# Row fetches from part of an expert loop, a gate product with its operands swapped, and four first tiles

## The reference

```python
x = attn_out.transpose(0, 2, 1, 3).reshape(B * S, H * D)          # 1536 x 512
logits = x @ w_gate
noisy = logits + np.log1p(np.exp(x @ w_noise)) * noise             # first mixture
top2 = np.argpartition(-noisy, 2, axis=1)[:, :2]                   # second: argmax(x @ w_gate)
...
h = np.maximum(x[mask] @ w1[e], 0.0)
out[mask] += top2_w[mask, k, None] * (h @ w2[e])                   # second: out[mask] = gate_w * ye
```

## Time and profile before

| | |
|---|---|
| three runs | 977.11, 982.68, 984.29 us, median 982.68 |
| the profiled execution | 984.25 us, its span 982.4 |
| busy | PE 857.7, PEld 727.2, DVE 601.8, ACT 356.4, POOL 412.4 us |
| mean granted clock of TensorE | 0.948 of full speed |
| stores of result tiles, both mixtures | 44 |
| chain that ended last | `DMA x_sb<-ys,pos 1%; POOL x_sb L568 1%; DVE x_sb L1133 0%; POOLq L53 0%` |
| L817, a reduction of 768 contiguous values to one, mean | 953 ns |
| ys<-stage 1024 KB, xs<-stage 512 KB, median to landing | 7.5, 5.5 us |

### The profile page before, as it was taken

One profiled execution on the slowest core, in us unless ns is written; L12 is line 12 of the kernel. 1 busy time (PEld: TensorE's weight loads), 2 busy tenths in 40 slices (PEclk: granted clock), 3 DMA queues, 4 the chain that ended last, 5 costly groups with the idle time before them and its releaser, 6 DMA issues. The chain is left out here.

```text
span 982.4 us, 17214 instructions
## 1 busy us (share of the span) xinstructions
PE 857.7 (87%) x4650; PEld 727.2 (74%) x4651; DVE 601.8 (61%) x1109; ACT 356.4 (36%) x597; POOL 412.4 (42%) x282
## 2 busy tenths in 40 slices
PE   4899999999984679999999999999566999999970
PEld 3788888888874568888888888887345888888860
DVE  5899999999986744444444444444475444444432
ACT  2677777777874114211111111101240344332000
POOL 3010101101040789643434343408747899885004
PEclk9999999999998598999999999999795999999995
DMA  6577659658685568442524252416674678773107
GB/s 146 125 205 203 148 156 242 181 120 219 187 295 199 176 251 257 169 164 91 165 88 168 89 167 94 162 65 209 205 231 171 213 249 252 231 248 109 43 33 257
DMA packets 100201, 171.46 MB, mean 175 GB/s; under 512 B 35600, under 2 KB 37648, under 8 KB 100176
## 3 DMA queue, kind: packets, MB, share of 16 engines
q1 hardware_dynamic: 66992, 82.79, 28.6%
q10 hardware_dynamic: 26944, 67.90, 21.4%
q0 software_dynamic: 6240, 20.45, 6.4%
HBM read 98.18 MB, written 53.48 MB: 154 GB/s over the span
## 5 line engine op out<-in xcount | busy, mean ns | idle before, releaser
L532 POOL TENSOR_TENSOR wring<-stage,wring 128x1024 f32 (+1 forms) x124 | 293.0, 2402 | 195.6 <-ACT wring L711 171.0
L711 ACT ACTIVATE wring<-stage 128x1024 f32 (+1 forms) x120 | 125.3, 1059 | 419.1 <-POOL wring L532 190.2
L1346 PE MATMUL bank<-wring,xT_hl 128*128 x352 | 144.0, 409 | 5.2 <-DVE xT_hl L1042 5.2
L1363 PE MATMUL bank<-wring,hT_hl 128*128 x352 | 142.7, 405 | 3.2 <-DVE hT_hl L1068 3.2
L1075 DVE COPY work<-bank 128x512 f32<-128x512 f32 x44 | 30.5, 693 | 181.0 <-PE bank L1365 171.3
L1348 PE MATMUL bank<-wring,xT_hl 128*128 x352 | 139.8, 397 | 0.0
L1347 PE MATMUL bank<-wring,xT_hl 128*128 x352 | 139.2, 395 | 0.0
L1365 PE MATMUL bank<-wring,hT_hl 128*128 x352 | 138.6, 394 | 0.0
L1364 PE MATMUL bank<-wring,hT_hl 128*128 x352 | 138.1, 392 | 0.0
L1056 DVE TENSOR_SCALAR work<-bank 128x512 f32<-128x512 f32 x88 | 60.9, 692 | 106.7 <-PE bank L1348 106.7
L516 POOL TENSOR_TENSOR wring<-raw,ones 128x192 fp32r<-128x192 f32 x32 | 15.5, 506 | 224.9 <-PE bank L1197 218.5
(11 more groups left out here) (173 smaller groups left out, 1356.3 us busy)
## 6 DMA issues: line engine op xcount, KB each, us to landing
stage<-in_moe_w_dram ACTq DMA_DIRECT2D x128, 512.0 KB, 3.9
wring<-wring SPq DMA_DIRECT2D x92, 192.0 KB
ys<-work SPq DMA_DIRECT2D x44, 256.0 KB, 3.6
work<-xs SPq DMA_DIRECT2D x40, 256.0 KB, 3.4
xs<-stage SPq DMA_DIRECT2D x7, 1024.0 KB, 4.8
ys<-stage SPq DMA_DIRECT2D x7, 1024.0 KB, 7.5
xs<-stage SPq DMA_DIRECT2D x7, 512.0 KB, 5.5
raw<-in_q_dram SPq DMA_DIRECT2D x16, 192.0 KB, 4.1
```

The lines of the kernel that those rows point to most:

```text
L532: nc.gpsimd.tensor_tensor(wring[:, bass.ds(at + DC * F, GW)], stage[:, at_stage(g, j), :], wring[:, bass.ds(at, GW)].bitcast(F32), ALU.sub ...
L711: nc.scalar.activation(wring[:, bass.ds(parity * SLOT + high_at(j), GW)], stage[:, j % STAGES, :], ACT.Copy).then_inc(w_high, 1)
L1346: mm(o, xT_hl[:, 0, c, :], wh, start=c == 0, stop=False)
L1363: mm(y_ps[:], hT_hl[:, 0, c, :], wh, start=c == 0, stop=False)
```

## The change

- The loads of constants on SP go behind the first head's puts.
- `lg_heads` is laid out with the head as the last index; both result buffers are cleared whole, a part in each round.
- `FIRST` is 4: four tiles are fetched directly from the tokens, at other places among the scatters.
- VectorE computes a table `need[m]`: for each token tile the number of sorted tiles whose results must be stored before its rows of the last expert can be fetched. `fetch_high` reads it before each fetch and waits for that many stores. For the first mixture eight tiles of rows go to `stage` and four to `work`, the latter after the last store.
- So that `stage` is free, ScalarE and POOL prepare only the first four pieces of the second mixture's expert 0 ahead; the other four are loaded while tiles are mixed, and VectorE splits them (`second_low`) as in the first mixture. Low parts 0 to 3 of expert 1 move into `sort_rows(1)`, ahead of scatter 7, the other four stay behind the scatters.
- The low rows are scaled by ScalarE; the gate weights are computed inside `experts`; the last scaling and the output stores are ScalarE's.
- The gate product has the turned rows as the stationary operand and the 8 gate columns moving; its result needs no turning back. Ten idle products more (`keep_busy(10)`) follow TensorE's counts.

```diff
-    FIRST = 3
+    FIRST = 4
@@ SP, start
+            sp.wait_ge(prep_ev, 2)
+            put(q_hl[0], D, D, qk_rest, 0)
+            put(k_lb[0], 0, D, qk_rest, D)
+            put_bits(0, 0)
+            load_qk(1)
             for r in range(2):
                 for at, w in ((D, moe_w_gate), (D + E, moe_w_noise)):
...
-                clear_y(0, i * share[0], share[0])
+                    clear_y(m, i * share[m], share[m])
...
-            clear_y(1, NTMIN[1], NT[1] - NTMIN[1])
+                clear_y(m, NT[m] - rest[m], rest[m])
@@ POOL
-                fetch_at = ((2, 6, 10), (2, 5, 8))[m]
+                fetch_at = ((1, 5, 7, 9), (1, 4, 5, 6))[m]
                 for t in range(TT):
                     if m == 1:
                         pool.wait_ge(mixed, t + 1)
+                        if t == 7:
+                            pool.wait_ge(w_low, (E + 1) * GRAN)
+                            low_part(E + 1, 1, range(GRAN // 2))
...
-            def fetch_rows(m):
-                pool.wait_ge(y_st, 16 * (T0[m] + NT[m]))
...
-                for t in range(TT):
-                    if t >= GOT:
-                        pool.wait_ge(mixed, m * TT + t - GOT + 1)
-                    fetch_one(y_got[t % GOT] if m == 0 else rows_of(t), m, TOPK[m] - 1, t, y_back[t % GOT])
+            def fetch_high(m):
+                for t in range(TT):
+                    if m == 0 and t >= EARLY:
+                        stored = pool.value_load(tiles_upto[0][0:1, E - 1:E], min_val=NTMIN[0], max_val=NT[0])
+                    else:
+                        stored = pool.value_load(need[m][0:1, t:t + 1], min_val=NTMIN[m] // E, max_val=NT[m])
+                    pool.wait_ge(y_st, stored * 16 + T0[m] * 16)
+                    pool.sem_inc(y_seen, 1)
+                    fetch_one(y_got(t) if m == 0 else rows_of(t), m, TOPK[m] - 1, t, y_back[t])
...
             pool.wait_ge(rt_tab, 1)
+            low_part(E, 0, range(GRAN // 2))
             fetch_low()
-            low_part(E, E % 2)
-            fetch_rows(0)
-            low_part(E + 1, 1, range(3))
+            pool.wait_ge(w_low, E * GRAN + GRAN // 2)
+            fetch_high(0)
             sort_rows(1)
-            low_part(E + 1, 1, range(3, GRAN))
+            low_part(E + 1, 1, range(GRAN // 2, GRAN))
@@ ACT
-            high_part(1, 0, E, 0, table(0, E - 2))
+            high_part(1, 0, E, 0, table(0, E - 2), range(GRAN // 2))
+            act.wait_ge(rt_gate, 1)
+            act.wait_ge(y_low, 16 * TT)
+            for t in range(TT):
+                nc.scalar.activation(x, x, ACT.Copy, scale=gatew[0][:, t:t + 1]).then_inc(low_scaled, 1)
             for t in range(TT):
                 act.wait_ge(rt_T, t + 1)
                 nc.scalar.activation(route_T(1, t), route_xT[t % 2][:], ACT.Copy).then_inc(rt_Tc, 1)
+                if t in (2, 4, 6, 8):
+                    act.wait_ge(mixed, t)
+                    load_piece(1, 0, GRAN // 2 + t // 2 - 1)
+            for j in range(GRAN // 2, GRAN):
+                second_high(j)
...
+            for t in range(TT):
+                act.wait_ge(y_back[t], 32)
+                nc.scalar.activation(x, x, ACT.Copy, scale=gatew[0][:, t:t + 1]).then_inc(out_rdy, 1)
+                act.wait_ge(out_rdy, t + 1)
+                act.dma_start(ot[t // QT, t % QT], x_sb[:, t // QT, t % QT]).then_inc(out_st, 16)
@@ DVE
-                vec.tensor_copy(tiles_upto[m][:], cum[0:1, :]).then_inc(rt_tab, 1)
+                link(vec.tensor_copy(tiles_upto[m][:], cum[0:1, :]))
+                link(vec.tensor_tensor(last_tiles[0:1], bc(last_seen[0:1], [1, TT, TT], 2), bc(steps128[0:1], [1, TT, TT], 1),
+                                       ALU.is_gt))
+                link(vec.tensor_reduce(last_seen[0:1], last_tiles[0:1], AX.X, ALU.add))
+                vec.tensor_scalar(need[m][:], last_seen[0:1], cum[0:1, E - 2:E - 1], None, ALU.add).then_inc(rt_tab, 1)
...
-                link(vec.tensor_scalar(x, x, gatew[0][:, t:t + 1], None, ALU.mult))
-                vec.scalar_tensor_tensor(out=x, in0=y_got[t % GOT], scalar=gatew[1][:, t:t + 1], in1=x,
+                vec.scalar_tensor_tensor(out=x, in0=y_got(t), scalar=gatew[1][:, t:t + 1], in1=x,
...
                 hT_split(0)
+                gate_weights(m)
@@ PE
-                    ins = mm(lgT_ps[t % 2], wg_sb[:, c, :], xt[:, c * P:(c + 1) * P], start=c == 0, stop=c == DC - 1)
-                ins.then_inc(rt_lgT, 1)
-            def turn_logits(t):
...
+                    ins = mm(lg_ps[:, t * E:(t + 1) * E], xt[:, c * P:(c + 1) * P], wg_sb[:, c, :],
+                             start=c == 0, stop=c == DC - 1)
+                ins.then_inc(rt_lg, 1)
```

161 lines of the change are left out of this document (78 added, 83 removed).

## The result

The changed kernel takes 973.26 us (median of 6 runs, 970.48 to 974.99) against 981.62 for the kernel before (6 runs, 977.11 to 984.29): a ratio of 0.9933, 95% interval 0.9909 to 0.9956. That is 8.4 us where the forecast summed up 19.8, though 973.3 lies inside the stated range of 956 to 975. The profiled execution took 972.41 with a span of 970.6, so against the profiled 984.25 the difference is 11.8.

The account below looks back on a forecast made before the run. TensorE is full inside both expert loops, so only the seams (start, first experts, between mixtures, end) can move. Terms sum to -19.8 from the profiled 984.25, giving 964.45, or 962.9 as a median; 8 in 10 range 956 to 975.

Parts of the forecast that it names:

- Start, -1.0: Kernel start: constants' loads behind the first puts bring TensorE's first scores 1.0 us earlier, bounds 0 and 3.9.
- Attention, -0.5: Attention: head sums laid out for contiguous reduction, 0.95 instead of 1.45 us, save 0.5; added clears cost nothing.
- First experts, -5.6 net of the chain: First mixture: a fourth first tile removes the wait for scatters, up-product 5.6 us earlier despite 2.2 longer routing; POOL late next.
- Mixing, -10.7: Between the mixtures: mixing starts earlier and a tile costs TensorE 1.57 instead of 1.71 us, saving 10.7.
- rival (d): Mixing: turned gate product bound by loads on a slow clock, 5.4 us a tile, kernel slower at 1009; 4%.
- The rule of the Trainium skill: Gate product in mixing: load time goes with stationary columns, some 10 us added, mixing about -1, median 972; not followed.
- Routing, -3.8: Second mixture's routing chain: two 128x96 VectorE operations return to 0.26 us with POOL idle, saving 3.8.
- Trainium skill's rule on operations with two inputs in SBUF: Second routing: VectorE tensor_tensor with both inputs in SBUF and GpSimd reading SBUF lock each other out; 2.29 against 0.26.
- POOL afterwards, +6.8 and +3.0: Second mixture's fourth up-product: TensorE waits 6.8 us more for weights from POOL, then starts cold, 3 more.
- The end, -8.0: Kernel end: ten of twelve row fetches need only the second-last store, saving 8.0 us, bounds -10 and -4.

Follow-up runs that it names:

- old_start: Changed kernel with the constants' loads ahead of the first puts again and only the last seven result tiles of the second mixture cleared; 0.9995 of the kernel before.
- first pair: The original profiled executions of the kernel before and the changed kernel, neither altered; 984.25 against 972.41 us.
- second pair: Both kernels unaltered, traced again on a chip without TensorE's idle times; changed 973.86 against 978.19 us before, ratio 0.9950.
- third pair: Both kernels unaltered, traced again on a chip where both show TensorE's idle times; changed 989.61 against 987.15 us before, ratio 1.0031.
- wide80: Changed kernel with the eight gate columns repeated ten times as moving operand, 80 columns a pass; 0.9891 and, once more, 0.9876 of the kernel before.
- narrow_busy: Changed kernel with four idle products of 128 columns behind each mixed tile's transposes and narrow gate product; 0.9969 of the kernel before.
- early_w: Changed kernel with 80 gate columns, expert 0's deferred half split during mixing, VectorE making expert 1's first four low parts; 957.88 us, ratio 0.9805 to the kernel before.
- late_end: Changed kernel with the second mixture's last twelve row fetches each waiting for the last result tile; ratio 1.0086.
- late_mix: Changed kernel with all twelve fetches of the first mixture's last expert waiting for the last stored tile; ratio 1.0073.

## Why the forecast was wrong

- **Start, -1.0:** right for the first scores, 0.7 to 1.3, and `old_start` gives that back. It does not carry to the first counts by itself (315.9 without it, 316.0 with it, at the same clock).
- **Attention, -0.5:** the head sum fell from 1.43 to 0.95 us as forecast. The first pair has 2.8 more, the second none. The forecast left out TensorE's clock in the first and last head: all three traces of the kernel before have it low in a part of both, nine of sixteen with the changed start in neither, and the 4 us between those traces go with it.
- **First experts, -5.6 net of the chain:** the way was right and the size too in the second pair (-5.3), with POOL late next as named. In the first pair it is -3.5: behind the 2.09 us wait for POOL the step takes 13.9 us instead of 12.3, with a granted clock of 0.89 from 365 to 380 against 1.00 in the second pair. The term had no room for this. In four of the six comparisons TensorE also has idle times of its own in that stretch and the stage gains 1 us, less than its longer chain costs (third pair); the trace of the kernel before that the forecast had shows none.
- **Mixing, -10.7: the step that failed.** Its first half held: the first mixed transposes come 5.7 us after the last down-product. Even so it was TensorE's sequencer, stepping over unused steps, that ended that wait, and not the first mixed row. The second half failed: "a tile costs 1.57" took the passes from a row with 80 columns at the high clock, and the sum took for granted that the clock rises after three tiles as it did with 128 columns. It did not rise: the granted clock is 0.50 throughout, 2.455 a tile, 29.9 us instead of 21. That is 8.9 us; the profiled execution is 8.0 off the forecast, and that the two are so near is in part luck, as the clocks in attention (2.8 to the good) hide what the first experts (2.1) and the first half here (0.9) fell short. With the clock up the price was wrong the other way: `wide80` has 1.29 a tile, 0.43 for the transposes where the forecast took 0.59. The forecast had this as rival (d), priced at 5.4 a tile with no load hidden behind a pass and given 4%. The clock half of that rival came true and the load half did not: a pass at the low clock is 0.196, not 0.54. I tied two doubts together that are independent, and gave the pair the chance of both at once. A rival "low clock alone", 12 times 0.885 above the forecast, would have read 973.5.
- The rule of the Trainium skill (TensorE: Matmul & The Clock Gate, section LDWEIGHTS) gave a median of 972, near the 973.3 measured, but that is a coincidence. With the clock up, `narrow_busy` has 0.10 for a load of 128 columns and its pass together, near the 107 ns that the page's formula gives for the load, and that is less than the 0.12 of the 128-column passes it replaces. Passes of 80 columns take 0.11, so nearly the same, from which I read that the loads set the pace of a narrow product; they cost nothing against the product before until the clock is low.
- **Routing, -3.8:** right, 2.9 to 3.3; the 128x96 operations are at 0.26 with POOL idle, after 2.29 and 2.00 beside its low parts. That agrees with the Trainium skill's rule on operations with two inputs in SBUF (SBUF — State Buffer, section Who interferes with whom). The gate-weight operation that takes 2.44 beside POOL's low parts (2.25 and 1.90 in the other pairs) has one such input, so that rule doesn't account for it, and its two neighbours, at 0.24 and 0.23, weren't held up.
- **POOL afterwards, +6.8 and +3.0:** right, 6.2 to 7.2 and 2.1 to 2.7, and `early_w`, where the wait is gone, shows that they were the queue on POOL.
- **The end, -8.0:** right, 8.0 to 8.8; `late_end` gives 7 of it back. At the mixing the early fetches are worth 7, by `late_mix`.

## What to carry to other kernels

When an edit makes TensorE's passes narrower, price them at both levels of its clock, and ask of every stretch that follows an idle time whether the new work will bring the clock up. Padding the moving operand with columns that nobody reads cost 0.05 us in eight passes here and took the stage from 29.9 to 18.1 us. Keep two independent doubts as two rivals. A wait in a stretch where the engine has idle times of another kind on some chips was worth removing only on the others. And when traces of one kernel differ, look at the granted clock of each stretch before calling the difference spread.

## What the runs showed of the hardware

- Eight passes with 128x128 stationary: 0.81 us with 8 moving columns and 0.86 with 80 at the high clock, 1.57 with 8 at the low one. A stage in which TensorE was busy all but 0.04 of 29.93 us with the narrow passes, and with transposes between, stayed at the low level to its end, in eight traces of eight. With 80 columns the clock rose in seven of seven, 3.6 to 11.9 us after the first transposes.
- TensorE showed idle times of 0.2 to 2.4 us between matmuls, ending with nothing that the trace shows, in its third step of the first mixture: in all fourteen traces of four comparisons, one of them of the kernel before, and in none of the six traces of the two others. They ended within five microseconds of POOL's last scatter. That its instructions arrive late behind those transfers is argued from this, not shown.
- In the first and the last head of attention the same code ran with the granted clock at 1.00 in some traces and at 0.91 and 0.94 in others, and the first counts came at 312 or at 316 us accordingly.
